# Finding the first slot's rows from one rank column, with reordered routing work around the end of attention

## The reference

```python
# attention: 2 x 8 heads, 768 rows, head size 64, 4 sink keys + a window of 128
scores = scale * np.matmul(q, k.transpose(0, 1, 3, 2)); keep = is_sink | in_window
a = softmax(np.where(keep, scores, -1e9)); x = (a @ v)          # -> [1536, 512]

# mixture of experts: 8 experts, 512 -> 1024 -> 512, the two best per token
noisy_logits = x @ w_gate + np.log1p(np.exp(x @ w_noise)) * noise
top2, top2_w = two best experts of a token and their softmax weights
for e in range(8):
    for k in range(2):
        mask = top2[:, k] == e
        h = np.maximum(x[mask] @ w1[e], 0.0)
        out[mask] += top2_w[mask, k, None] * (h @ w2[e])

# a dense layer with mish: 512 -> 2048 -> 512
h = x @ w_in
g = h * np.tanh(np.where(h > 20.0, h, np.log1p(np.exp(np.minimum(h, 20.0)))))
return g @ w_out
```

## Time and profile before

| | |
|---|---|
| median of 3 runs | 784.29 us (783.91 to 784.30) |
| the profiled execution | 783.87 us |
| its span, first to last instruction | 781.8 us |
| PE busy | 760.9 us, 97% of the span |
| DVE, ACT, POOL busy | 515.4, 285.4, 314.2 us |
| chain that ended last, by engine | PE 87%, DVE 6%, issue 3%, ACT 2%, POOL 1% |
| granted TensorE clock, mean | 0.989 of full speed |

### The profile page before, as it was taken

One profiled execution on the slowest core, in us unless ns is written; L12 is line 12 of the kernel. 1 busy time (PEld: TensorE's weight loads), 2 busy tenths in 40 slices (PEclk: granted clock), 3 DMA queues, 4 the chain that ended last, 5 costly groups with the idle time before them and its releaser, 6 DMA issues.

```text
span 781.8 us, 13281 instructions
## 1 busy us (share of the span) xinstructions
PE 760.9 (97%) x4228; PEld 627.1 (80%) x4229; DVE 515.4 (66%) x905; ACT 285.4 (37%) x594; POOL 314.2 (40%) x331
## 2 busy tenths in 40 slices
PE   8999969999999999999999999989999999999997
PEld 5888757888888888888888888768888888888886
DVE  6789965545445454544545445468998888878876
ACT  6888713030303003030030300356555554545443
POOL 5599936673833708337083918511020020000000
PEclk9999979999999999999999999999999999999999
DMA  6475574644532615417153624010000110010001
GB/s 208 159 252 177 158 235 138 200 161 136 187 123 75 222 38 180 128 64 231 41 176 119 200 96 122 29 54 29 28 27 28 55 54 1 1 54 1 1 0 55
DMA packets 49486, 82.87 MB, mean 106 GB/s; under 512 B 18080, under 2 KB 22240, under 8 KB 49440
## 3 DMA queue, kind: packets, MB, share of 16 engines
q10 hardware_dynamic: 13600, 33.96, 13.2%
q1 hardware_dynamic: 31440, 33.89, 13.1%
q0 software_dynamic: 4400, 14.42, 6.6%
HBM read 66.01 MB, written 16.25 MB: 105 GB/s over the span
## 4 chain that ended last, share of the span: by engine, by line
PE 87%; DVE 6%; issue 3%; ACT 2%; POOL 1%; another core or an unknown queue 1%; DMA 0%; DVEq 0%; ACTq 0%; POOLq 0%
PE bank L1345 21%; PE bank L1356 21%; PE bank L1420 16%; PE bank L1401 15%; PE bank L1329 4%; PE bank L1235 2%; PE bank L1322 2%; PE bank L1210 2%; PE bank L1219 1%; PE bank L1244 1%; PE bank L1194 1%; PE bank L1393 1%; DVE x_sb L887 0%; DMA xg<-x_dram,first_idx 0%
## 5 line engine op out<-in xcount | busy, mean ns | idle before, releaser
L577 POOL TENSOR_TENSOR wgt<-stage,wgt 128x1024 f32 (+1 forms) x64 | 151.2, 2402 | 101.2 <-ACT wgt L738 101.2
L1356 PE MATMUL bank<-wgt,hT 128*128 (+1 forms) x744 | 185.3, 398 | 0.0
L1345 PE MATMUL bank<-wgt,xT 128*128 (+1 forms) x744 | 182.6, 394 | 0.0
L1345 PEld LDWEIGHTS bank<-wgt,xT 128*128 128x128 f32 x744 | 137.3, 188 | 27.5 <-DVE xT L1039 0.2
L738 ACT ACTIVATE wgt<-stage 128x1024 f32 (+1 forms) x64 | 61.6, 1045 | 265.0 <-PE bank L1356 252.0
L1356 PEld LDWEIGHTS bank<-wgt,hT 128*128 128x128 f32 x744 | 135.2, 188 | 25.3
L1420 PE MATMUL bank<-wgt,gT 128*128 128x512 f32 x576 | 141.3, 395 | 4.8 <-DVE gT L1137 4.8
L1401 PE MATMUL bank<-x2T,wgt 128*128 128x512 f32 (+1 forms) x588 | 138.1, 385 | 0.9 <-DVE x2T L1114 0.9
L1420 PEld LDWEIGHTS bank<-wgt,gT 128*128 128x128 f32 x576 | 108.4, 190 | 28.7 <-DVE gT L1137 6.1
L1401 PEld LDWEIGHTS bank<-x2T,wgt 128*128 128x128 f32 x588 | 108.6, 188 | 23.0 <-POOL wgt L651 1.1
L1083 DVE TENSOR_SCALAR h<-bank 128x512 f32<-128x512 f32 x62 | 42.9, 692 | 60.7 <-PE bank L1345 56.5
(11 more groups left out here) (174 smaller groups left out, 935.5 us busy)
## 6 DMA issues: line engine op xcount, KB each, us to landing
stage<-in_moe_w ACTq DMA_DIRECT2D x48, 512.0 KB, 3.4
stage<-in_moe_w SPq DMA_DIRECT2D x16, 512.0 KB, 5.4
y_dram<-y_sb SPq DMA_DIRECT2D x31, 256.0 KB
stage<-in_moe_w_in ACTq DMA_DIRECT2D x8, 512.0 KB, 4.0
stage<-in_moe_w_out ACTq DMA_DIRECT2D x8, 512.0 KB, 4.1
v_in<-in_v SPq DMA_DIRECT2D x8, 384.0 KB
x_dram<-x_sb SPq DMA_DIRECT2D x16, 192.0 KB, 2.7
out<-o_sb SPq DMA_DIRECT2D x12, 256.0 KB, 2.0
```

Source lines behind the costliest of these rows:

```text
L577: nc.gpsimd.tensor_tensor(cols(parity, 1, u * UNIT, UNIT), stage[:, u, :], cols(parity, 0, u * UNIT, UNIT).bitcast(fp32), ALU.subtract).th ...
L1345: ins = T.matmul(HA[half][:], xT[:, a, c, :], cols(par, b, c * F + half * 512, 512), start=c == 0 and n == 0, stop=c == NC - 1 and n == 2)
L1356: ins = T.matmul(YB[kk % 2][:], hT[:, a, c, :], cols(par, b, NC * UNIT + c * DM, DM), start=c == 0 and n == 0, stop=c == F // P - 1 and n ...
```

## The change

Eight edits, all between the sixth pair of heads and slot 0's first products, apart from the earlier start of POOL's weight parts.

1. Slot 0's rows come from expert 0's column of `c` and of the ranks: `first_tok` = `c`'s column times the token number, `first_rank` = the rank column out of the accumulator, `first_row_hot` compares it with the ramp. 6 products per group instead of 12, and no picking of ranks ahead of them. `rank_rows` is cut in two; the slots' `row_hot` matrices are made later, two of the four behind `first_idx`.
2. PE's first rank product of a group waits for `c` alone and not for its running sum.
3. Ahead of the last gate sums DVE adds three of the four finished pairs' parts of group 1 for the last two tiles and stores the sum in their place, so that the last sum adds 3 parts per gate and not 8.
4. DVE's routing of group 0 is spread over more steps of attention.
5. POOL's weight parts start at unit 10 and take three of five units, before at 14 and three of four. SP issues the loads of expert 0's weights ahead of that pair's `v` load and x store.
6. The ramp is stored 6 wide (768 numbers a row) and not 24 wide (3072), and made four units earlier.
7. A dummy gather: SP stores a small tensor, POOL gathers it behind its last piece of attention work and waits for it.
8. Slot 0 alone: x is rounded on ACT, and PE runs the eight passes on rounded x and then the four on the rest, for the first half.

```diff
-        WEIGHTS_FROM = 14
+        WEIGHTS_FROM, WEIGHT_UNITS, WEIGHT_PARTS = 10, 5, (0, 1, 3)
@@ SP: the loads of expert 0's weights move ahead of load_v and store_x
                     load_qk(i + 1, (i + 1) % 2)
+                for u in range(2 * (i - 2), min(2 * (i - 1), UNITS)):
+                    src, to = unit_of(0, u)
+                    sp.dma_start(to, src).then_inc(unit_loaded[u], 16)
                 sp.wait_ge(pv_ready, QT * (i - 1))
                 load_v(i, i % 2)
                 store_x(i - 2)
...
+                    sp.dma_start(spare_dram, ident[:, 0:8]).then_inc(spare_stored, 16)
@@ POOL
-                if n == PROBS - 2:
+                if n == PROBS - QT:
                     pool.wait_ge(qk_ready, 4 * NP)
-                    nc.gpsimd.tensor_copy(ramps[:], ramp[:].unsqueeze(2).broadcast_to([P, P, 2 * NT])).then_inc(ramps_ready, 1)
+                    nc.gpsimd.tensor_copy(ramps[:], ramp[:].unsqueeze(2).broadcast_to([P, P, QT])).then_inc(ramps_ready, 1)
...
+            pool.wait_ge(spare_stored, 16)
+            nc.gpsimd.indirect_dma_start(out=spare_row[:], out_offset=None, in_=spare_dram,
+                                         in_offset=bass.IndirectOffsetOnAxis(ap=spare_idx[:, 0:1].bitcast(u32), axis=0)
+                                         ).then_inc(spare_read, 16)
+            pool.wait_ge(spare_read, 16)
             pool.wait_ge(x_stored, 16 * 2 * NP)
             pool.wait_ge(first_routed, 1)
             gather(0, 0)
@@ ACT, behind the exp of the score gaps
+            act.wait_ge(x_transposed, 1)
+            nc.scalar.activation(xT[:, 0], bank[2][:].rearrange("p (c s) -> p c s", c=NC), ACT.Copy).then_inc(xT_rounded, 1)
@@ DVE, new functions
+            def sum_pairs(first, count):
+                dve.wait_ge(x_ready, QT * (NP - 1))
+                parts = x_sb[:, first:first + count, PPB:NP - 1, :, D:VW].rearrange("p t i h c -> p t c (i h)")
+                held = rt["cut"][:, 0:count * GL].rearrange("p (t c) -> p t c", t=count)
+                after(V.tensor_reduce(held, parts, AX.X, ALU.add))
+                after(V.tensor_copy(x_sb[:, first:first + count, NP - 2, 1, D:VW], held))
...
+            def first_expert(g):
+                after(V.tensor_tensor(first_tok[:, js], of_group("c", g)[:, 0:QT], tok_f[:, js], ALU.mult))
+            def first_ranks(g):
+                dve.wait_ge(ranks_ready, g + 1)
+                after(V.tensor_copy(first_rank[:, g * QT:(g + 1) * QT], RANKS[g][:, 0:QT]))
+            def first_rows_hot(g):
+                V.tensor_tensor(first_row_hot[:, :, js], ramps[:], first_rank[:, js].unsqueeze(1).broadcast_to([P, P, QT]),
+                                ALU.is_equal).then_inc(first_rows_ready, 1)
@@ DVE, steps u of attention
+                if u == PROBS - 2 * QT - 2:
+                    noisy_gates(0)
                 if u == PROBS - 2 * QT:
-                    noisy_gates(0)
                     pick_max(0, 0, rt3["lg"][:, 0:QT])
+                if u == PROBS - 2 * QT + 2:
                     pick_first(0, 0)
+                if u == PROBS - QT - 2:
+                    hide_best(0)
                 if u == PROBS - QT:
-                    hide_best(0)
                     pick_max(0, 1, by_token("cut"))
+                if u == PROBS - QT + 2:
                     pick_first(0, 1)
@@ DVE, the drain
             norm_step(PROBS - 6, 2)
+            sum_pairs(4, 2)
             gate_sums(1, 0, 2)
-            rows_hot(0)
...
             gate_sums(1, 2, 2)
+            rows_hot(0, 0)
             norm_step(PROBS - 2, 1)
             norm_step(PROBS - 1, 1)
-            gate_sums(1, 4, 2).then_inc(sums_ready, 1)
+            sum_last(4, 2).then_inc(sums_ready, 1)
+            first_rows_hot(0)
@@ PE
+                pe.wait_ge(chosen_ready, g + 1)
+                T.matmul(RANKS[g], not_earlier[:], of_group("c", g), start=g == 0, stop=False)
                 pe.wait_ge(counts_in, g + 1)
-                T.matmul(RANKS[g], not_earlier[:], of_group("c", g), start=g == 0, stop=False)
                 T.matmul(RANKS[g], ones[:], of_group("inc", g), start=False, stop=True).then_inc(ranks_ready, 1)
...
+                if isinstance(t, int) and t == 0:
+                    pe.wait_ge(xT_rounded, 1)
+                    up_by(MM3[0:2], True)
+                    pe.wait_ge(xT_ready, 1)
+                    up_by(MM3[2:3], False).then_inc(up_done, 1)
```

More of the change, by code:

```diff
@@ L137, in attention_moe_mish @@
                        ("oh", 2 * E * NT), ("m1", NT), ("m2", NT), ("gap", NT), ("s1", NT), ("c", E * NT), ("inc", E * NT),
-                       ("own", 2 * NT), ("begin", 2 * NT), ("ns", E), ("incn", E), ("excn", E), ("sel", 2 * E * NT),
+                       ("begin", 2 * NT), ("ns", E), ("incn", E), ("excn", E), ("sel", 2 * E * NT),
                        ("p01", 2 * NT), ("den", NT), ("tab", 32 * (E - 1)), ("ex", 32)):
@@ L145, in attention_moe_mish @@
     a_h = route.tensor("a_h", [P, 2 * NT], f16)
-    first_hot = route.tensor("first_hot", [P, 2 * NT], f16)
+    first_tok = route.tensor("first_tok", [P, NT], f16)
+    first_rank = route.tensor("first_rank", [P, NT], f16)
     r_h = route.tensor("r_h", [P, 2 * NT], f16)
@@ L441, in _ @@
                 store_x(i - 2)
-                for u in range(2 * (i - 2), min(2 * (i - 1), UNITS)):
-                    src, to = unit_of(0, u)
-                    sp.dma_start(to, src).then_inc(unit_loaded[u], 16)
                 if i == NP - 1:
                     sp.wait_ge(consts_ready, 1)
+                    sp.dma_start(spare_dram, ident[:, 0:8]).then_inc(spare_stored, 16)
                     for t in range(FULL, SLOTS):
@@ L907, in gate_sums, with sum_last @@
                 return V.tensor_reduce(lgs[:, g * QT + first:g * QT + first + count, :], parts, AX.X, ALU.add)
+            def sum_pairs(first, count):
[4 more added lines that the diff above has]
+                after(V.tensor_copy(x_sb[:, first:first + count, NP - 2, 1, D:VW], held))
+            def sum_last(first, count):
+                dve.wait_ge(x_ready, PROBS)
+                parts = x_sb[:, first:first + count].rearrange("p t i h c -> p t (i h) c")[:, :, 2 * NP - 3:2 * NP, D:VW]
+                return V.tensor_reduce(lgs[:, QT + first:QT + first + count, :], parts.rearrange("p t a c -> p t c a"), AX.X, ALU.add)
             def noisy_gates(g):
@@ L948, in first_expert @@
             def first_expert(g):
[L949 removed]
+                js = slice(g * QT, (g + 1) * QT)
+                after(V.tensor_tensor(first_tok[:, js], of_group("c", g)[:, 0:QT], tok_f[:, js], ALU.mult))
[3 more added lines that the diff above has]
+            def first_rows_hot(g):
+                js = slice(g * QT, (g + 1) * QT)
+                if g == 0:
+                    dve.wait_ge(ramps_ready, 1)
+                V.tensor_tensor(first_row_hot[:, :, js], ramps[:], first_rank[:, js].unsqueeze(1).broadcast_to([P, P, QT]),
+                                ALU.is_equal).then_inc(first_rows_ready, 1)
             def rank_rows(g):
@@ L1036, in split_xT @@
                 src = bank[2][:].rearrange("p (c s) -> p c s", c=NC)
-                V.tensor_copy(xT[:, 0], src).then_inc(xT_rounded, 1)
+                if not (isinstance(t, int) and t == 0):
+                    V.tensor_copy(xT[:, 0], src).then_inc(xT_rounded, 1)
                 dve.wait_ge(xT_rounded, t + 1)
@@ L1289, in first_rows @@
             def first_rows(g):
-                pe.wait_ge(rows_ready, 2 * g + 2)
-                for w in range(2):
-                    for j in range(g * QT, (g + 1) * QT):
-                        m = w * NT + j
-                        ins = T.matmul(FIRST_IDX, row_hot[w][:, :, j], first_hot[:, m:m + 1].broadcast_to([P, 2]),
-                                       start=m == 0, stop=m == 2 * NT - 1)
+                pe.wait_ge(first_rows_ready, g + 1)
+                for j in range(g * QT, (g + 1) * QT):
+                    ins = T.matmul(FIRST_IDX, first_row_hot[:, :, j], first_tok[:, j:j + 1].broadcast_to([P, 2]),
+                                   start=j == 0, stop=j == NT - 1)
                 return ins
@@ L1347, in up, with up_by @@
                     return ins
+                def up_by(products, begins):
+                    for c in range(NC):
+                        for n, (a, b) in enumerate(products):
+                            ins = T.matmul(HA[0][:], xT[:, a, c, :], cols(par, b, c * F, 512), start=begins and c == 0 and n == 0,
+                                           stop=not begins and c == NC - 1)
+                    return ins
                 def down(k0, k1):
```

57 lines of the change are left out of this document (34 added, 23 removed).

## The result

The changed kernel takes 780.39 us (median of 5 runs, 779.22 to 781.13) where the kernel before takes 784.3 beside it (5 runs): ratio 0.9943, 95% interval 0.9929 to 0.9957. On two other chips it came to 0.9926 [0.9908, 0.9944] and 0.9932 [0.9911, 0.9954]. The forecast was 781.4, so 2.9 us of gain; measured are 3.9 by the two medians and 4.5 by the ratio (5.3 to 5.8 on the other chips). By the ratio the kernel would take 779.8 us where the one before takes 784.3, just under the stated range of 779.9 to 783.5. It is faster, and more so than forecast, though the profile shows a good part of a still larger gain lost again.

What follows compares the result with a forecast made beforehand. PE was taken to bound the kernel, with a chain of waits over the drain before slot 0 at 122.07 us. Terms -0.23 - 1.90 - 0.62 + 0.17 - 0.3 = -2.88 gave 781.4 us, range 779.9 to 783.5.

Steps and rivals of the forecast that it cites:

- attention's term of the sum: Attention, the moved routing, weight parts and ramp: totals of work unchanged, only PE's hole closes partly, -0.3 us.
- T to H: From the end of `rt_c` to the end of the one-hot matrix that `first_rows` needs: 3.83 becomes 1.93, -1.90 us.
- hole at 70 to 80 us: PE's 1.3 us gap in attention, from group 0's six operations at one step; closes by 1.3 at best.
- These were not awaited: Attention's last cuts on POOL: freeing them of the ramp's 3072 numbers gains nothing, as the chain has no POOL there.
- Locks: Attention rival: moved two-input DVE operations meeting POOL's cost 1.06 us each; chance 0.12 for part loss, 0.07 for slower.
- price of three locks: Attention: three more DVE meetings with POOL cost +3.2 against -2.58 for the rest, giving 784.9 us, slower than before.
- case of two: Attention: two more DVE meetings with POOL turn the -0.3 into +1.8, giving 783.5 us.
- H to the transposes: From the one-hot matrix's end to slot 0's transposes: fewer products and a quicker gather, 5.70 becomes 5.08, -0.62 us.
- rival of a late gather: Ahead of slot 0: x lands 1.3 us late and holds the first gather, 0.9 lost, 782.3 us; chance 0.12.
- The dummy gather: Ahead of the first real gather: shortens its start by 0.62 and its issue by 0.20 us, only 0.44 worth anything.
- The clock: Transposes to slot 0: PE's clock rises late, so 0.35 us of `INDEX` runs at the lower level, +0.17.
- the forecast's other case: Transposes to slot 0: clock back ahead of the transposes gives about -0.45 instead of +0.17, and a sum of -3.5.

Runs made afterwards that it cites:

- parts and loads: The kernel before with only POOL's weight parts started at unit 10, three in five units, and expert 0's weight loads issued earlier: 783.1 us, 0.9971.
- four kernels built on the one before: The kernel before with one piece of the change: spread alone (0.999), loads alone (1.0), parts alone (1.0047), parts and loads (0.9971).
- spread alone: The kernel before with only DVE's routing of group 0 spread over more steps of attention: 784.84 us, 0.999.
- loads alone: The kernel before with only SP's loads of expert 0's weights issued ahead of the `v` load and the x store: 785.48 us, 1.0.
- `warm(20)`: The changed kernel with 20 idle products on PE instead of 10 ahead of slot 0: 778.43 us, 0.9918.
- fills moved with `warm(13)`: The changed kernel with y_dram's fills issued behind x's last store and the first gather's landing, and 13 idle products, not 10: 777.59 (0.9909) and 777.91 us (0.9905).
- no spread: The changed kernel with group 0's routing back in three bundles behind three units instead of seven: 778.47 us (0.9904), again 777.41 us (0.9899).
- parts alone: The kernel before with only POOL's weight parts from unit 10, three of five units, without the earlier loads: 787.96 us, 1.0047.
- fills moved: The changed kernel with SP's fills of y_dram issued behind x's last store and the first gather's landing: 778.66 us, 0.991.
- no dummy: The changed kernel without the dummy gather and the small store that feeds it, on two chips: 777.8 us (0.9899) and 778.73 us (0.9915).
- late ramp: The changed kernel with POOL's narrow ramp written at unit PROBS - 2 again instead of PROBS - QT: 779.56 us, 0.9935.

## Where the prediction was right, and where it failed

The step that failed is the attention's term of the sum, -0.3, with its premise that DVE's total stays the same: measured are -4.15, and DVE's busy time in attention fell by 5.8 us (85.23 to 79.42) with the two halves of edit 5 and nothing else. Behind it two terms went the other way that the sum had at a gain and at nothing, the wait for x and the clock in slot 0. That the two profiled executions differ by 2.74 us, near to the forecast 2.88, is errors cancelling and no merit of the sum.

- **T to H: right.** 1.94 us measured, 1.93 forecast. DVE's piece fitted inside the rank products, the cast stands right behind them. `first_idx` came at H + 0.85 (forecast 0.96).
- **Edit 3: right in kind.** The last sum takes 0.26 (forecast 0.25). The 0.10 charged for the matrix ahead of the norms was not seen: DVE idles 0.32 between it and the norms.
- **Attention: the step that failed.** The prediction put -0.3, because "the total is the same" for DVE and for POOL's 24 parts, and the hole at 70 to 80 us "can close by 1.3 at best". It measured -4.15: -2.35 from edit 5 (99.84 to 97.49), about -1.2 from the narrow ramp and what stands with it (to 96.29), 0 to -0.6 from edit 4. The total was not the same: with edit 5 DVE's differences for q and k took 18.47 us instead of 23.59, as fewer of them met a subtraction of POOL (3 and not 8). The earlier trace rows had DVE at 9.71 and 9.42 of 10 and POOL at 9.51 and 9.44: the engines that bounded these steps were in the row I used, and I read the row for PE. "Earlier weight loads have their units ready earlier: nothing" failed with it: alone they are nothing, and without them the parts cost 2.3. "These were not awaited" is open: in the kernel with parts and loads the chain runs through the ramp's cast and the cuts, in the kernel before it does not.
- **Locks: they came the other way.** The case of the earlier trace rows (0.21 becoming 1.27) did not return in the changed kernel; the longest operation of group 0's picking behind 70 us took 0.69. The Trainium skill, "SBUF — State Buffer", section "Who interferes with whom", was read as speaking against edit 4; the attention of the changed kernel is 0 to 0.6 us shorter with the edit than without. What the rule speaks of did bear on the time, but in operations that the prediction left out of its count, DVE's differences for q and k, and through edit 5, which took meetings away. The prediction's price of three locks, 784.9, also drops the -0.3 that its case of two keeps; with it the price is 784.6, and still slower.
- **H to the transposes: the rival of a late gather came true, at a chance of 0.12.** It had x level with `first_idx` and priced x 1.3 late; x was 1.50 behind `first_idx` (110.54, 109.04). The forecast for this stretch, -0.62, became +0.85: 1.47 lost where the rival had 0.9, as POOL began the gather 0.74 behind x's landing. The attention term's failure fed this: last sums 3.34 us sooner, while x's landing came only 1.75 sooner (112.29 to 110.54), as x's stores stand in SP's queue behind what it issues from 86 us on. "It stays full, so the order inside it moves no end" was right of the queue's end and wrong of x, which sits at that end.
- **The dummy gather.** Taken as 0.62 + 0.20, measured 0.12 + 0.3 to 0.5. With it x lands 1.3 to 1.6 us later, which takes more than that back; the store that feeds it explains 0.6 of this.
- **The clock.** Forecast: 0.35 us of `INDEX` at the lower level, +0.17. Measured: the clock had risen by 112.05, ahead of the transposes, and the stretch took 0.66 less than before, 0.3 of it by edit 8. In the four kernels built on the one before the clock was back ahead of the transposes too, and the stretch took 2.17 without edit 8, 0.45 less than before, as the forecast's other case had it. The Trainium skill, "TensorE: Matmul & The Clock Gate", section "What's actually happening", says that the moment of the rise varies; the rises lay 3.86 us behind H in the first trace of the changed kernel and 4.21 and 4.39 in the two others, so it agrees. In the kernel before the rise lay 6.71 behind H, in the four built on it 3.6 to 5.2: that the one trace of before had so late a rise is luck. Then the clock fell again behind the pause, and the slots took 2.21 more. Part of that may be luck of the one trace of before too: in the kernels with the spread alone and the loads alone, which don't touch this place, the clock fell behind 0.49 and 0.69 us and the slots took 386.03 and 385.27. The sum had nothing for this, and the rival of the late gather priced PE's wait at its length only.
- **Edit 8: right that `INDEX` and not the rest of x releases slot 0 in the changed kernel**, but its price wasn't nothing: undone it costs 0.3.
- **The mish part: +0.79.** Its low-clock stretch was 6.83 us where it was 3.42. In two other profiles of the same changed kernel it was 3.41 and the part took 276.0, so the change doesn't explain it; the profiled execution drew the longer one.

The best of these kernels is the changed one with edit 4 left out, 777.41 us (0.9899), or with the fills moved and 13 idle products, 777.91 (0.9905); these two can't be told apart. A kernel with both was not run.

## What to carry to other kernels

Read engines' work per step of the pipeline, not over ten microseconds: helper engines that are 94 to 97% busy on average were most likely the bound in single steps here, while the main engine still looked 99% busy. And don't take an engine's total as fixed when another's work moves: here DVE's fell by 5.8 us because POOL's parts met fewer of its operations. Edits that move work earlier have to be tried together with what feeds them; alone, each of the two here was worth nothing or less. And when a drain is shortened, follow every transfer that the next stage needs back to the head of its queue: here x's landing was set by fills issued 24 us before, of a tensor that no gather reads for another 380 us.

## What the hardware showed that I had not expected

- A pause of PE can cost more than its length, as the granted clock fell to 0.50 behind many of them. The table has every profile of this study. The length alone doesn't decide: the clock fell behind 0.49 us, and not behind 0.84.

| PE's pause ahead of the transposes, us | profiles | lower clock behind it, us | the slots, us |
|---|---|---|---|
| 0.07 | `warm(20)`; fills moved with `warm(13)`, twice | none | 383.75; 384.34 twice |
| 0.23, 0.25, 0.29 | no spread; parts alone; the kernel before | none | 383.46, 384.31, 383.75 |
| 0.46, 0.53 | fills moved; no spread again | none | 383.83, 383.81 |
| 0.49, 0.69 | spread alone; loads alone | 3.41 | 386.03, 385.27 |
| 0.84 | parts and loads | none | 383.96 |
| 0.71 to 1.54 | no dummy, twice; changed kernel, twice; late ramp | 3.41 | 384.87 to 385.22 |
| 1.64, 1.98 | edit 8 undone; changed kernel, first trace | 6.83 | 385.96 twice |

- A two-input operation of DVE that began beside POOL's subtraction took 1.65 us where it took 0.77 without one, and the subtraction 1.58 instead of 1.27.
- POOL's cast of 3072 numbers a row took 2.74 us, of 768 numbers 0.82.
- The first indirect gather took 1.15 us to issue in the kernel before and the four built on it, 1.48 in the changed kernel without the dummy gather (twice), and 0.95 once a dummy had run.
